# Weight items in four places, loads cut into pieces between the stores, and the first unit's weights split ahead of the attention

## The reference

```python
# q, k, v: (8, 8, 576, 64); all float32
kv  = einsum('bhsd,bhse->bhde', k, v)
out = einsum('bhsd,bhde->bhse', q, kv)
out = out / sqrt(mean(out*out, -1) + 1e-6) * g_norm
x   = out.transpose(0, 2, 1, 3).reshape(4608, 512)
x   = (sigmoid(x @ w_gate) * (x @ w_val)) @ w_mid      # 512 -> 1536 -> 512
h   = x @ w_in                                         # 512 -> 2048
y   = where(h > 0, h, exp(min(h, 0)) - 1) @ w_out      # 2048 -> 512
```

## Time and profile before

| | |
|---|---|
| median of 3 runs | 1816.13 us (1812.59 to 1821.2) |
| profiled execution, its own time | 1814.1 us |
| its span, first to last instruction | 1812.3 us |
| PE busy | 1684.3 us (93%) |
| DVE / ACT / POOL busy | 1182.8 / 843.3 / 185.2 us |
| mean granted TensorE clock | 0.968 |
| HBM read / written | 191.89 / 145.75 MB |

### The profile page before, as it was taken

The page is one execution under the profiler, slowest core; times in us unless marked ns, Lnnn a source line. Parts: engine busy times, 40 slices in busy tenths (PEclk is TensorE's granted clock), DMA queues, the critical chain, the costliest instruction groups (busy, mean ns, idle before and its releaser), DMA issues.

```text
span 1812.3 us, 27151 instructions
## 1 busy us (share of the span) xinstructions
PE 1684.3 (93%) x10536; PEld 1655.4 (91%) x10536; DVE 1182.8 (65%) x1429; ACT 843.3 (47%) x1283; POOL 185.2 (10%) x185
## 2 busy tenths in 40 slices
PE   7996977879898889999999999999999889999999
PEld 6885977879898889999999989999999889999999
DVE  4778855657455656557767767676766666766674
ACT  6784543445334444434444445455544434434442
POOL 4654222112002110000000000000000000000000
PEclk9997998999999999999999999999999989999999
DMA  9894376565856653484343492333246843343332
GB/s 262 247 277 140 138 270 244 222 225 210 332 202 224 228 215 148 181 323 148 140 140 140 164 349 94 142 140 139 105 144 230 326 158 118 123 159 124 120 122 75
DMA packets 187544, 339.33 MB, mean 187 GB/s; under 512 B 11552, under 2 KB 147744, under 8 KB 186528
## 3 DMA queue, kind: packets, MB, share of 16 engines
q1 hardware_dynamic: 187424, 337.69, 52.9%
HBM read 191.89 MB, written 145.75 MB: 186 GB/s over the span
## 4 chain that ended last, share of the span: by engine, by line
PE 65%; DMA 11%; DVE 6%; issue 5%; ACT 4%; SPq 1%; POOL 0%; ACTq 0%; DVEq 0%; POOLq 0%
PE pair L875 32%; PE pair L940 19%; PE pair L908 14%; DMA weight_items<-out_w 7%; DVE s L1365 2%; DMA u_elu<-s 1%; DVE ring L1291 1%; DVE e L1470 1%; DMA u_gated<-ub 1%; DMA x_gated<-s 1%; DMA raw<-u_elu 1%; ACT e L1165 1%; ACT s L1096 1%; ACT e L1194 1%; ACT ring L1061 1%
## 5 line engine op out<-in xcount | busy, mean ns | idle before, releaser
L875 PE MATMUL pair<-ring,wreg 128*128 128x384 f32 x5040 | 913.2, 342 | 87.3 <-ACT s L1096 66.9
L875 PEld LDWEIGHTS pair<-ring,wreg 128*128 128x128 f32 x5040 | 900.4, 193 | 99.7 <-ACT s L1096 71.4
L940 PE MATMUL pair<-wreg,ring 128*128 128x256 f32 x3024 | 365.9, 284 | 11.4 <-ACT s L1219 10.6
L940 PEld LDWEIGHTS pair<-wreg,ring 128*128 128x128 f32 x3024 | 365.4, 193 | 11.9 <-ACT s L1219 10.8
L1365 DVE TENSOR_TENSOR s<-s,pair 128x768 f32<-128x768 f32 (+1 forms) x252 | 210.9, 837 | 215.8 <-PE pair L875 168.8
L908 PE MATMUL pair<-ring,wreg 128*128 128x384 f32 x1512 | 262.2, 334 | 0.0
L908 PEld LDWEIGHTS pair<-ring,wreg 128*128 128x128 f32 x1512 | 262.1, 188 | 0.0
L1291 DVE TENSOR_TENSOR ring<-raw,ring 128x1024 fp32r<-128x1024 f32 (+1 forms) x162 | 180.5, 1133 | 110.4 <-ACT ring L1071 93.2
L1165 ACT ACTIVATE e<-e 128x768 f32<-128x768 f32 x72 | 61.0, 847 | 162.3 <-DVE e L1470 162.3
L1071 ACT ACTIVATE ring<-raw 128x1024 fp32r<-128x1024 f32 x108 | 111.7, 1051 | 40.6 <-DVE raw L1325 26.0
L1291 DVE TENSOR_TENSOR ring<-sum,ring 128x768 fp32r<-128x768 f32 (+1 forms) x90 | 90.0, 1014 | 17.6 <-ACT ring L1061 6.6
(11 more groups left out here) (99 smaller groups left out, 1488.8 us busy)
## 6 DMA issues: line engine op xcount, KB each, us to landing
weight_items<-out_w SPq DMA_DIRECT2D x98, 512.0 KB, 2.7
raw<-u_elu SPq DMA_DIRECT2D x18, 2048.0 KB, 8.2
u_gated<-ub SPq DMA_DIRECT2D x144, 192.0 KB, 2.5
u_elu<-s SPq DMA_DIRECT2D x72, 384.0 KB, 2.4
wreg<-weight_items SPq DMA_DIRECT2D x7, 3584.0 KB, 12.7
wreg<-weight_items SPq DMA_DIRECT2D x49, 512.0 KB, 7.1
x_raw<-x_attention SPq DMA_DIRECT2D x12, 1536.0 KB, 6.6
raw_k<-u_gated SPq DMA_DIRECT2D x6, 2304.0 KB, 8.2
```

The lines of the kernel that those rows point to most:

```text
L875: mm = pe.matmul(dst[:, g, 0:NT], w[:, a, cols], ring[:, slot, b, kt, :], start=(i in STARTS and kt == a == b == 0), stop=(kt == 1 and a = ...
L940: mm = pe.matmul(dst[:, 0, 0:256], s[:, b, 2 * c + kt, :], w[:, a, cols], start=(i in STARTS and c == kt == a == b == 0), stop=(c == 3 and ...
```

## The change

1. Stored weight items have four places: two in `out_w` and two more in a new tensor `out_x` at 69 KiB. ACT waits for the store of the item four before. `o`, `qt`, `kv`, `rms` of the attention change places in memory with `qk`.
2. SP's order is new. x loads are cut into four transfers, two at a time; unit loads into seven; the load of a super tile of `u_elu` into two. A function `between(n, at)` places them between the stores of unit n. Loads of weight chunks move to the unit of a visit that stores no weights (j = 2).
3. Chunk 0 is loaded before the first heads and split in the first steps of the attention, no longer in the last ring. Products P6 and P5 of unit 0 stand between the last steps that multiply by the norm factors; ACT and DVE no longer wait for the stores of the attention before unit 0 (ACT does before chunk 2).
4. ELU: ACT takes the snapshot of P1 before the Exp of the preceding unit's c21, which had come first.
5. Out: the sums S3, S2, S1 stand at items 3, 4, 5 (before 1, 2, 4) and S4 at item 0 of the next unit (before 6).

```diff
-                 ("qk", [SP_, QK, 2, RT, 2, D], F32, buf_at(0)),
+                 ("o", [P, RING, S], F32, buf_at(0)),
+                 ("qt", [P, 2, S], F32, buf_at(0) + RING * S * 4),
+                 ("kv", [P, 2, P], F32, buf_at(0) + (RING + 2) * S * 4),
+                 ("rms", [P, HN], F32, buf_at(0) + (RING + 2) * S * 4 + KIB),
...
+                 ("qk", [SP_, QK, 2, RT, 2, D], F32, buf_at(3)),
...
+            ("out_x", [P, 2, 2, 512], F32R, 69 * KIB),
...
+        def out_slot(c, i):
+
+            ring_at = stored(c, i) % 4
+            return out_x[:, ring_at - 2] if ring_at >= 2 else staging(c)[2][:, ring_at]
...
-            def load_unit(c, b):
-
-                wait_chunk_stored(sp, c)
-                sp.dma_start(wreg[:, 7 * b:7 * b + 7].rearrange("p i a c -> p i (a c)").bitcast(F32),
-                             wt_dram[c - DIRECT]).then_inc(s_wld[b], 16)
...
+            def load_unit_items(c, b, items):
+                for i in items:
+                    load_cell(7 * b + i, c, i)
+
+            def load_mid_cells(b, cells):
+                for cell in cells:
+                    load_cell(7 * b + cell, MID + (7 * b + cell) % 3, (7 * b + cell) // 3)
+
+            def load_out_cells(b, cells):
+                for cell in cells:
+                    at = (7 * b + cell - 21) % 28
+                    load_cell(7 * b + cell, OUT + at % 4, at // 4)
+
+            def load_x(src, sup, tiles=range(4)):
+                for kt in tiles:
+                    sp.dma_start(x_raw[:, kt, :], src[kt * P:(kt + 1) * P, sup * SUPER:(sup + 1) * SUPER]).then_inc(
+                        s_xld, 16)
...
+                for kh in halves:
+                    sp.dma_start(raw4[vis % 2][:, 8 * kh:8 * kh + 8, :],
+                                 u2_dram[1024 * kh:1024 * kh + 1024, vis * 2 * TT:(vis + 1) * 2 * TT].rearrange(
+                                     "(k p) t -> p k t", p=P)).then_inc(s_r4[vis % 2][kh], 16)
...
+            load_chunk(0)
             for r in range(QR):
                 load_pair(0, r)
-            load_chunk(0)
...
+            load_chunk(2)
             wait_attention_over(sp)
...
+            def between(n, at):
+
+                vis, j = n // HALF1, n % HALF1
+                if j == 0 and vis < LAST_B:
+                    if at == 0:
+                        sp.wait_ge(s_lo, split1(vis, P4))
+                    if at < 2:
+                        load_x(x1_dram, (vis + 1) % NS, (2 * at, 2 * at + 1))
+                if j == HALF1 - 1 and at < 2:
+                    for c, when in ((3, (2, 0)), (4, (2, 1)), (5, (5, 0)), (6, (5, 1)), (7, (8, 0)), (8, (8, 1)),
+                                    (9, (11, 0)), (10, (11, 1)), (11, (14, 0)), (12, (20, 0)), (13, (20, 1)),
+                                    (14, (23, 0)), (15, (23, 1)), (16, (26, 0))):
+                        if (n, at) == when:
+                            if c == SECOND_STAGING:
+                                sp.wait_ge(s_prod, prod(unit1(LAST_A, 2), P4))
+                            load_chunk(c)
+                pieces = ((0, 1, 2), (3, 4), (5, 6), ())[at]
+                if n == unit1(LAST_A, 1):
+                    if at == 0:
+                        sp.wait_ge(s_wlo, ITEMS * SECOND_STAGING)
+                        wait_chunk_stored(sp, SECOND_STAGING - 1)
+                    load_unit_items(3, BUF1[3], pieces)
+                if n == unit1(LAST_A, 2):
+                    if at == 0:
+                        sp.wait_ge(s_prod, prod(n - 1, P4))
+                    load_unit_items(4, BUF1[4], pieces)
+                if n == unit1(NS, 0) and at > 0:
+                    load_unit_items(5, BUF1[5], ((0, 1, 2, 3), (4, 5, 6), ())[at - 1])
+                if n == unit1(LAST_B - 1, 1):
+                    if at == 0:
+                        sp.wait_ge(s_wlo, ITEMS * CHUNKS)
+                        wait_chunk_stored(sp, CHUNKS - 1)
+                    load_mid_cells(0, pieces)
+                if n == unit1(LAST_B, 0):
+                    if at == 0:
+                        sp.wait_ge(s_lo, split1(LAST_B, P4))
+                        wait_gated(0)
+                        load_k0(0)
+                    if at == 2:
+                        load_a22(0)
+                if n == unit1(LAST_B, 1):
+                    if at == 0:
+                        sp.wait_ge(s_prod, prod(n - 1, P4))
+                    load_mid_cells(1, pieces)
+                if n == unit1(LAST_B, 2):
+                    if at == 0:
+                        sp.wait_ge(s_prod, prod(n, P1))
+                        load_a12(0)
+                    else:
+                        load_mid_cells(2, ((0, 1, 2), (3, 4), (5, 6))[at - 1])
...
-                for c, at in ((2, 0), (3, 1), (4, 3), (5, 4), (6, 6), (7, 7), (8, 9), (9, 10), (10, 12), (11, 13),
-                              (12, 18), (13, 19), (14, 22), (15, 24), (16, 25)):
...
+                store_weight(n, 0)
+                between(n, 0)
+                store_weight(n, 1)
                 store_gated(n, "11")
+                between(n, 1)
                 for i in (2, 3, 4):
                     store_weight(n, i)
                 store_gated(n, "22")
+                between(n, 2)
                 store_weight(n, 5)
                 store_gated(n, "12")
                 store_weight(n, 6)
                 store_gated(n, "21")
+                between(n, 3)
...
+                    load_unit_items(IN + 1, BUF3[1], range(4))
                     store_x2(n, "22")
+                    load_unit_items(IN + 1, BUF3[1], range(4, ITEMS))
...
+                    if j == 1 and at == 0 and last:
+                        load_raw4(0)
+                    if j > 0 and at == 0 and last:
+                        sp.wait_ge(s_prod, prod(n - 1, P4))
+                    if j == 2 and at == 0 and last:
+                        load_raw4(1, (0,))
+                    pieces = ((0, 1), (2, 3), (4, 5), (6,))[at]
+                    if n < FIRST3 + 2:
+                        load_unit_items(IN + 2 + n - FIRST3, BUF3[2 + n - FIRST3], pieces)
+                    if last and j > 0:
+                        load_out_cells(BUF3[j - 1], pieces)
...
+            load_out_cells(BUF3[3], range(4))
+            for c in range(2):
+                sp.wait_ge(s_st[c], 16 * FIRST4)
+            load_raw4(1, (1,))
+            load_out_cells(BUF3[3], range(4, 7))
...
+            weight_sums(0)
...
-            static_steps(step, PAIRS + 1, PAIRS + LB - NP)
+            static_steps(step, PAIRS + 1, PAIRS + 3)
             pe.wait_ge(s_o_sb, 2 * PAIRS)
             pe.wait_ge(s_sqhi, 2 * PAIRS)
             gated_product(0, P2)
-            static_steps(step, PAIRS + LB - NP, PAIRS + LB)
+            static_steps(step, PAIRS + 3, PAIRS + 4)
             gated_product(0, P6)
+            static_steps(step, PAIRS + 4, PAIRS + 5)
             pe.wait_ge(s_kv_sb, 2 * PAIRS)
             pe.wait_ge(s_rms, B)
-            for i in range(P5, ITEMS):
+            gated_product(0, P5)
+            static_steps(step, PAIRS + 5, PAIRS + LB)
+            for i in range(P7, ITEMS):
                 gated_product(0, i)
...
-                if c >= DIRECT and stored(c, i) >= 2:
-                    act.wait_ge(s_wst[stored(c, i) % 2], 16 * (stored(c, i) // 2))
+                if c >= DIRECT and stored(c, i) >= 4:
+                    act.wait_ge(s_wst[stored(c, i) % 4], 16 * (stored(c, i) // 4))
...
+                if c == 1 and i == 0:
+                    act.wait_ge(s_kv_ps, PAIRS)
                 if c == 2 and i == 0:
-                    act.wait_ge(s_kv_ps, PAIRS)
+                    wait_attention_over(act)
...
-                fill3(n, 0)
                 act.wait_ge(s_prod, prod(n, P1))
                 act.wait_ge(s_st[0], 16 * n)
                 if n == FIRST3:
                     act.wait_ge(s_sum, summed(2, NS - 1, "S4"))
                 act.activation(s1[:, :, :], pa[:, :, 0:NT], ACT.Copy).then_inc(s_snap, 1)
+                if n > FIRST3:
+                    exp_c21(n - 1)
+                fill3(n, 0)
                 fill3(n, 1)
                 exp(n, 0, e0)
...
+            def exp_c21(n):
+
+                act.wait_ge(s_neg, n - FIRST3 + 1)
+                act.activation(e_3[1][:, :, :], e_3[1][:, :, :], ACT.Exp, scale=-1.0).then_inc(s_exp, 1)
...
+            split_weight(0, P1)
+            split_weight(0, P2)
+            for p in range(2 * RING):
+                static_steps(step, p, p + 1)
+                if p < 5:
+                    split_weight(0, P6 + p)
             looped_steps(act, step, 2, TRIPS - 1)
...
+                for i in {PAIRS - 1: (P1, P2), PAIRS: (P6,), PAIRS + 2: (P5,), PAIRS + 3: (P7,), PAIRS + 4: (P3,),
+                          PAIRS + 5: (P4,)}.get(p, ()):
+                    split_x1(0, i)
+            act.wait_ge(s_ms, PAIRS)
+            act.wait_ge(s_rlo, B)
...
-                    name = {1: "S3", 2: "S2", 4: "S1", 6: "S4"}.get(i)
```

(4 more changed lines are left out.)

199 lines of the change are left out of this document (56 added, 143 removed).

## The result

After the change the kernel takes 1719.1 us (median of 4 runs, 1715.57 to 1719.34) beside 1814.4 us (4 runs, 1809.11 to 1821.2; the three above and one more): a ratio of 0.947 (95% interval 0.943 to 0.950). Faster was predicted, with 1712 us and a range of 1690 to 1738. The profiled execution has a span of 1716.8 us, 95.5 us less than before.

The account below looks back on a forecast made before the run. The bound of units 3 to 29 was taken to be the stores' place in the transfer queue, with two places for items as the reach. -95 - 1 + 1 - 9 = -104 gave 1712 us, range 1690 to 1738.

Parts of the forecast that it names:

- Stores of weight items: Units 3 to 29: with four places and moved loads, weight splits no longer wait for stores; -95 of 99.5 us.
- rival 1: Transfers can't follow: mixed traffic at no more than 284 GB/s, only 71 us gained in units 3 to 29, 1736; chance 0.13.
- One sign: ACT's weight splits: no wait for `weight_items` above 10 us in all.
- Pieces: Loads cut into pieces, 114 transfers more: a piece costs nothing beyond its bytes.
- Rival 4: Slower, each piece pays for itself: 1.1 us per transfer, 114 more cost 125 us, 1837; chance 0.03.
- Start: First heads: chunk 0 landing ahead and seven ACT splits in the first steps make everything later; +4 us, between 0 and 8.5.
- my lower bound: Start of the kernel: 0 us lost, the heads catch up since the same bytes must be in by the fifth pair.
- End of the attention: P6 and P5 of unit 0 between factor steps, P7 at about 180.5 for 185.4: gain 5 us, between 0 and 8.
- The two together: Start and end of the attention summed: -1 us.
- ELU: ELU units: wait moves from P6 to P7, +4 to +5; first and last units get back about 4; sum +1 us.
- Rival 2: ELU and out lose all their waits: snapshot of P6 doesn't take P1's place, cells in time, 1695; chance 0.12.
- Out: First out unit: seven cells there some 20 us in, wanted at 15; some 5 of 14.2 us stay, -9.

Follow-up runs that it names:

- e1: Kernel before the change with the four places for stored weight items alone, loads whole and where they were: 1745.3 us (ratio 0.961).
- e2: Changed kernel with two places for stored weight items in place of four, everything else of the change kept: 1754.5 us (ratio 0.965).
- e9: Changed kernel with each of its 98 weight item loads cut in two by columns, both halves to all 128 partitions: 1719.7 us (ratio 0.946).
- e6: Changed kernel with chunk 0 loaded behind the first heads, and summed and split in the last eight steps as before: 1720.6 us (ratio 0.947).
- the ten: Ten profiles of kernels with both the early chunk 0 and the new end of the attention: unit 1 starts at 189.9 us on average (188.6 to 192.2).
- e7: Changed kernel with the old end of the attention (P6 and P5 of the first unit behind all factor steps), chunk 0 still early: 1716.6 us (ratio 0.945).
- e3: Changed kernel with ACT's old order in ELU units: Exp of c21 and first filling split ahead of the snapshot of P1: 1713.8 us (ratio 0.942).
- e5: Changed kernel with DVE's result of c21 moved behind the combine and minimum of the next ELU unit's 11: 1713.6 us (ratio 0.943).
- e8: Changed kernel with loads around the ELU units moved behind stores and started earlier: 1703.3 us (ratio 0.939).

## Why the prediction was right, and where it was off

- **Stores of weight items** (-95; -94.6). The mechanism and its size held. Both parts of the change carry it (e1, e2), which the prediction had not told apart. The rate was there: 279 GB/s over the stretch at a share of 0.76, and 395 to 400 where the queue was full, more than the 347 I went by, so rival 1 (284 GB/s at most) fell. The 347 was a mean over 10 us, in which pieces of 2 us went from 236 to 402 GB/s; it was never a limit. One sign was missed: I wrote at most 10 us of waits of the weight splits, and it is 16.5. A store lands 4.5 us after its issue in the median (2.7 in the earlier trace rows), so the places had more to cover than I reckoned. The stretch is 4.9 us over what is needed, 3.0 of it as waits of PE behind such splits; I had left 4.5.
- **Pieces** (0; 0). Rival 4 fell in e9: 98 more transfers on top cost nothing that the whole time shows. The Trainium skill's batches of at least 1 MiB ("DMA: Bandwidth & Descriptors", section Bandwidth; its table there is of transfers issued from GpSimd, and those here are issued by SP) did not matter for 512 KB transfers in one queue here: in unit 43, mixed with results of 384 KB, they moved 395 GB/s.
- **Start** (+4). The step that failed is that the later first heads stay late. They do come 5.4 us later (11.6 us of wait), but have caught up by the eighth pair, as my lower bound said. In addition seven splits and their sums no longer sit in the last eight steps, which I had costed at nothing: some 2 us gained (e6 against the ten).
- **End of the attention** (-5). The failed term is that P7 begins 4.9 us earlier and nothing behind it gets slower. The last write of `o` ended at 179.1, near my 178.5; but behind it I had only the combine, a sigmoid and the snapshot, and there also stands a weight split on DVE (179.03, 0.68 us) and one on ACT (181.04, 0.61 us), so P7 began at 182.4 and not at 180.5. And the three last products took 8.6 us and not 6.2, at a granted clock of 0.72, behind a wait that I had not counted. The gain is 1.4 us at most (e7).
- **The two together** (-1; -0.7). That they agree is luck twice over: two errors of opposite sign met (+4 was some -2, -5 was -1.4 at most), and the pair of profiles happens to lie close. The mean of the ten is 1.8 us ahead of the kernel before and 4.1 ahead of e1, which has the same attention.
- **ELU** (+1; +5.4). I had said 1.4, 0.6, 0.7 and 0 us for j = 3, 0, 1 and 2; it is 1.43, 0.54, 0.69 and 0. For j = 0 and 1 e3 and e5 show the chain that I read from the earlier trace rows. For j = 3 my chain lacked the split of the next x, which went behind the Exp with it: with the result out of the chain 1.27 of the 1.43 us remain (e5), so there the number came out and the reason is only in part mine. Rival 2 fell. The failed term is that the first and last units get back about 4: they lose 2.3 more (71.1 for 68.8 us), because the pieces stand ahead of results of 384 KB that a snapshot waits for (2.0 and 1.2 us in unit 43, 1.8 and 2.4 in unit 64, both for `u_elu`). With other places and an earlier start of the loads units 42, 43, 64 and 65 take 62.0 us (e8).
- **Out** (-9; -5.6). The mechanism was right, the seven cells. They came 22 us into the unit (1364.5), 20 predicted. The size was off by the wait in this unit, 6.8 us for 5, and by the low clock behind it (0.88 in the unit), which I had put at nothing.

Together the ELU and the out term make 7.8 of the 8.5 us between the -104 and the -95.5.

## What to carry to other kernels

When an engine waits for a store, look at what was issued ahead of it: more places to write to and an earlier place in the queue each brought more than half here, and overlap. At the other end, issue a load as soon as its buffer is free and behind the store whose landing somebody waits for next, not ahead of it (some 13 us here, with the same bytes in all; the two parts weren't told apart). Idle time that was moved to another product took the low clock with it here, and the products behind it paid (8.6 us for 6.2). Before an operation is moved behind another, follow both engines' programs to the next thing that the same engine has to deliver, since a wait that is taken away at one product tends to come up at the next.
